# Two chained MLPs: VectorE writes the activations of an up tile into SBUF in place of PSUM

## The chip, the cores and the metric

The kernel runs on one core of one Trainium2 chip. The metric is the device time of one execution in microseconds, lower is better. TensorE, VectorE (DVE), ScalarE (ACT), GpSimd (POOL) and SyncE (SP) each run their own list of instructions in order and meet at semaphores.

## The reference

The input is 2 x 4096 rows of 192 features. A mixing stage weights 7 neighbouring rows with a softmax, and then two MLPs follow, each 192 to 2048 to 192, without a bias:

```python
x = attn_out.reshape(B * S, D)          # softmax-weighted sum of 7 rows, per head
h = x @ w_in                            # first MLP: 192 -> 2048
g = np.maximum(0.01 * h, h)             # leaky ReLU
x = g @ w_out                           # 2048 -> 192
h = x @ w_in2                           # second MLP
g = np.where(h > 0.0, h, np.exp(np.minimum(h, 0.0)) - 1.0)   # ELU
out = g @ w_out2
```

All of it is in float32.

## The kernel before

**Numbers in two parts.** TensorE multiplies in the rounded type fp32r. To keep float32 precision each factor is split into a rounded part (`_hi`) and the rest (`_lo`), and three of the four products are made. ScalarE makes the rounded part with a copy that converts, and VectorE makes the rest with a subtraction.

**Tiles.** The 8192 rows are cut into 16 chunks of 512 rows (`T`). A phase is one MLP of one chunk. There are 32 of them, in the order of `run`: the first MLP of chunk c, the second MLP of chunk c-1, and so on. So the two MLPs alternate (m is 0 in the first, 1 in the second; c is the chunk; ph counts the phases; dm and dc name the phase before, whose down still runs). A phase has 8 steps (s; g counts them over all phases). A step makes 256 of the 2048 hidden features: two halves of 128 features by 512 rows, side by side in a tile of 128x1024.

**One step on its way through the engines:**
- TensorE, `up`: ten matmuls into `hidden[:, s % 2, :]`, in PSUM (two buffers of two banks). The semaphore `s_up` counts it.
- ScalarE writes `act[:, s % 2, :]`, in SBUF: 0.01 times hidden in the first MLP (L762); relu(-hidden), then exp of its negative, in the second (L765, L767). `s_act`.
- VectorE, `nonlinearity`: the maximum of the two, written back over `hidden` in PSUM (L894 in the first MLP, L897 in the second). `s_g`.
- ScalarE rounds it: `hid_hi` from `hidden` (L792). `s_hi`.
- VectorE takes the rest: `hid_lo` = `hidden` - `hid_hi` (L933). `s_lo`.
- TensorE, `down`: ten matmuls of `hid_hi` and `hid_lo` with the down weights `dn` into `y_a` and `y_b` (L524 to L531). `s_dn`.

`hidden`, `act`, `hid_hi` and `hid_lo` have two buffers each, chosen by s % 2. TensorE's order is up of step g, down of step g-2, up of g+1, down of g-1. Before up of step g it waits for `hid_lo` of step g-2 (`s_lo`), since that is the last reader of the PSUM buffer. Down of g-2 then needs no wait of its own.

**Work beside this.** GpSimd makes the mixing of a later chunk, `mixing`, from chunk 1 on: 7 products and 6 additions of 128x768, all from SBUF to SBUF (L281, L293). It starts when VectorE has finished the softmax weights of that chunk, in step 2 of a first-MLP phase. ScalarE and VectorE also split the inputs of a phase (L693, L695 and L858, L860 in steps 3 and 4 of a first-MLP phase; L677, L679 and L849, L851 in steps 5 and 6 of a second-MLP phase), transpose mixed and output chunks in 32x32 squares (L879, L889), and take y out of PSUM: in step 1 of a phase ScalarE copies y of the phase before (`ylow` and `ya`) and VectorE adds into `yb` (L874). TensorE waits for both (`s_ya`, `s_yb`) before the first down of the new phase, in step 2. In the first phases they also split the weights of both MLPs (L814, L341, L342).

The very first and the very last step are cut into halves (`step_by_halves`), with the same sequence.

Of the kernel before, what the change touches and what calls it, by code (L numbers as in the profile page):

```python
# [5 lines left out]
def attention_leaky_elu_mlps(  # L6
# [24 lines left out]
    f32 = mybir.dt.float32  # L31
    f32r = mybir.dt.float32r
    ALU = mybir.AluOpType
    ACT = mybir.ActivationFunctionType
# [31 lines left out]
    with ctx:  # L66
# [45 lines left out]
        act = sb("act", [P, 2, 2 * T], f32)  # L112
        zeros = act[:, 0, 0:T]
        hid_hi = sb("hid_hi", [P, 2, 2 * T], f32r)
        hid_lo = sb("hid_lo", [P, 2, 2 * T], f32r)
# [8 lines left out]
        hidden = ps("hidden", [P, 2, 2 * T])  # L124
# [32 lines left out]
        s_g = sem("hidden_ready")  # L157
        s_hi = sem("hidden_hi_ready")
        s_lo = sem("hidden_lo_ready")
# [5 lines left out]
        s_hi1 = sem("half_hidden_hi_ready")  # L165
# [49 lines left out]
        END = ST * LAST + ST - 1  # L215
# [8 lines left out]
        def signal(step_sem, half_sem, i):  # L224

            return step_sem if i else half_sem
# [27 lines left out]
        def known(c):  # L254
            return isinstance(c, int)
# [39 lines left out]
        def down_split(m, n):  # L295

            parts = DN_PARTS * m + n + 1
            return (s_dnlo, parts) if parts <= DN_POOL else (s_dnlov, parts - DN_POOL)
# [189 lines left out]
        def _(pe):  # L488
# [104 lines left out]
            def phase(m, c, ph, dm, dc):  # L593
                for s in range(ST):
                    g = ST * ph + s
                    if known(ph) and g == 0:
                        up_first()
                        continue
                    if s == 0:

                        pe.wait_ge(s_min if m else s_xin, 2 * (c + 1))
                    if known(ph) and ph == 0 and s % 2 == 0:

                        pe.wait_ge(s_uplo, s + 2)
                    if known(ph) and ph == 2 and s == 0:

                        pe.wait_ge(s_uplo, 4 * QUARTERS)
                    if not (known(ph) and ph == 0 and s < 2):

                        pe.wait_ge(s_lo, g - 1)  # L610
                    up(m, input_of(m, c), g, s)
                    if known(ph) and ph in (0, 2) and s in (2, 4, 6, 7):

                        pe.wait_ge(*down_split(m, (s - 1) // 2))
                    if s < 2:
                        if dm is not None:
                            down(dm, ST - 2 + s)
                    else:
                        if s == 2 and dm is not None:

                            pe.wait_ge(s_ya, ph)
                            pe.wait_ge(s_yb, ph)
                        down(m, s - 2)
                    if s == 6 and known(ph) and ph == 0:
                        transpose_mix(1)
# [14 lines left out]
        def _(act_e):  # L640
# [83 lines left out]
            def step_by_halves(m, g, s):  # L724
                if g == END:

                    act_e.wait_ge(s_g, END - 1)
                for i in (0, 1):
                    wait_half(act_e, s_up, s_up1, g, i)
                    a, h = act[:, s % 2, HALF[i]], hidden[:, s % 2, HALF[i]]  # L730
                    if m == 0:
                        nc.scalar.activation(a, h, ACT.Copy, scale=SLOPE).then_inc(signal(s_act, s_act1, i), 1)
                    else:
                        nc.scalar.activation(a, h, ACT.Relu, scale=-1.0).then_inc(signal(s_relu, s_relu1, i), 1)
                        act_e.wait_ge(signal(s_relu, s_relu1, i), ST * CH if i else 1)
                        nc.scalar.activation(a, a, ACT.Exp, scale=-1.0).then_inc(signal(s_act, s_act1, i), 1)
                if g == 0:
                    softmax_exp(1)
                if g == END:

                    act_e.wait_ge(s_dn, END - 1)
                for i in (0, 1):
                    wait_half(act_e, s_g, s_g1, g, i)
                    nc.scalar.activation(hid_hi[:, s % 2, HALF[i]], hidden[:, s % 2, HALF[i]], ACT.Copy).then_inc(signal(s_hi, s_hi1, i), 1)

            def phase(m, c, ph, dm, dc):
                for s in range(ST):
                    g = ST * ph + s
                    if halved(g):
                        step_by_halves(m, g, s)  # L750
                        if g == 0:
                            round_up(0, 2)
                        continue
                    if known(ph) and ph == 0 and s == 7:
                        mlp1_input_hi(1, 0)
                        mlp1_input_hi(1, 1)
                    act_e.wait_ge(s_up, g + 1)
                    if not (known(ph) and ph == 0 and s < 2):

                        act_e.wait_ge(s_g, g - 1)  # L760
                    if m == 0:
                        nc.scalar.activation(act[:, s % 2, :], hidden[:, s % 2, :], ACT.Copy, scale=SLOPE).then_inc(s_act, 1)  # L762
                    else:

                        nc.scalar.activation(act[:, s % 2, :], hidden[:, s % 2, :], ACT.Relu, scale=-1.0).then_inc(s_relu, 1)  # L765
                        act_e.wait_ge(s_relu, ST * c + s + 1)
                        nc.scalar.activation(act[:, s % 2, :], act[:, s % 2, :], ACT.Exp, scale=-1.0).then_inc(s_act, 1)  # L767
                    if s == 1 and dm is not None:
                        take_y(dm, dc, ph - 1)
                    if m == 1 and s in (5, 6) and not (known(c) and c >= CH - 2):  # L770
                        mlp1_input_hi(c + 2, s - 5)
                    if m == 0 and s in (3, 4) and not (known(c) and c == 0):
                        mlp2_input_hi(c - 1, s - 3)
                    if known(ph) and ph == LAST - 1 and s in (3, 4):
                        mlp2_input_hi(CH - 1, s - 3)
                    if m == 0 and s == 1 and not (known(c) and c in (0, CH - 1)):
                        softmax_exp(c + 1)
                    if known(ph) and g == 1:
                        round_up(0, 3)
                    if known(ph) and g in (2, 3, 4):  # L780
                        round_down(0, DN_POOL + g - 2)
                    if known(ph):
                        if (ph, s) in UP2_AT:
                            round_up(1, UP2_AT.index((ph, s)))
                        if (ph, s) in DN2_AT:
                            round_down(1, DN2_AT.index((ph, s)))

                    act_e.wait_ge(s_g, g + 1)
                    if not (known(ph) and ph == 0 and s < 2):

                        act_e.wait_ge(s_dn, g - 1)
                    nc.scalar.activation(hid_hi[:, s % 2, :], hidden[:, s % 2, :], ACT.Copy).then_inc(s_hi, 1)  # L792

            softmax_exp(0)
            round_up(0, 0)
# [10 lines left out]
        def _(dve):  # L806
# [84 lines left out]
            def nonlinearity(m, h, a, done):  # L891
                if m == 0:

                    nc.vector.tensor_tensor(h, h, a, ALU.max).then_inc(done, 1)  # L894
                else:

                    nc.vector.scalar_tensor_tensor(out=h, in0=a, scalar=-1.0, in1=h, op0=ALU.add, op1=ALU.max).then_inc(done, 1)  # L897

            def step_by_halves(m, g, s):
                for i in (0, 1):  # L900
                    wait_half(dve, s_act, s_act1, g, i)
                    nonlinearity(m, hidden[:, s % 2, HALF[i]], act[:, s % 2, HALF[i]], signal(s_g, s_g1, i))
                for i in (0, 1):
                    wait_half(dve, s_hi, s_hi1, g, i)
                    nc.vector.tensor_tensor(hid_lo[:, s % 2, HALF[i]], hidden[:, s % 2, HALF[i]], hid_hi[:, s % 2, HALF[i]].bitcast(f32),
                                            ALU.subtract).then_inc(signal(s_lo, s_lo1, i), 1)

            def phase(m, c, ph, dm, dc):
                for s in range(ST):
                    g = ST * ph + s  # L910
# [7 lines left out]
                        mlp1_input_lo(1, 1)  # L918

                    dve.wait_ge(s_act, g + 1)  # L920
                    h = hidden[:, s % 2, :]
                    nonlinearity(m, h, act[:, s % 2, :], s_g)
                    if known(ph) and g == 1:
                        split_up(0, 2)
                    if s == 1 and dm is not None:
# [4 lines left out]
                        softmax_b(c + 1)  # L930

                    dve.wait_ge(s_hi, g + 1)
                    nc.vector.tensor_tensor(hid_lo[:, s % 2, :], h, hid_hi[:, s % 2, :].bitcast(f32), ALU.subtract).then_inc(s_lo, 1)  # L933
                    if m == 1 and s == 2 and not (known(c) and c >= CH - 2):
                        turn_mix(c + 2)
                    if m == 1 and s in (5, 6) and not (known(c) and c >= CH - 2):
# [55 lines left out]
```

## Time and profile before

| | us |
|---|---|
| median of 3 runs | 1211.51 (1210.0 to 1213.1) |
| profiled execution, span | 1212.5 |
| TensorE matmuls busy | 1186.3 (98%) |
| VectorE busy | 814.6 (67%) |
| ScalarE busy | 745.8 (62%) |
| GpSimd busy | 354.3 (29%) |

The profiled execution's only time is its span, from its first to its last instruction. Each engine's busy time is the sum over its instructions. A "chain of waits" follows the work that ended last back to what released it. A table by stretches gives each engine's busy time in a part of the span, and the granted TensorE clock (1.00 is full). In a timeline a row is one instruction with its start and duration, and in square brackets the idle time of its engine before it and what ended that.

### The profile page before, as it was taken

The page shows a single profiled execution, that of the slowest core. Times are in us where ns is not written, and L with a number is a line of the kernel's source. Part 1 is how long each engine was busy: PE and PEld are TensorE (multiplying, and loading weights), DVE is VectorE, ACT ScalarE, POOL GpSimd, SP SyncE. Part 2 cuts the span into 40 slices and gives each one's busy share as a digit, 9 for nine tenths or more (in the row PEclk, how much of TensorE's full clock was granted, in tenths as well). Part 3 has the DMA queues.
Part 4 walks back from the last instruction along what each step waited for, and adds up shares of the span by engine and source line. Part 5 has one row for each costly group of instructions (what it writes and reads, how often), then busy time and mean ns, then how long its engine had stood idle before and what let it go on. Part 6 is the DMA issues. An engine that isn't in the chain of part 4 may idle for free.

```text
span 1212.5 us, 14538 instructions
## 1 busy us (share of the span) xinstructions
PE 1186.3 (98%) x5208; PEld 973.8 (80%) x5208; DVE 814.6 (67%) x778; ACT 745.8 (62%) x815; POOL 354.3 (29%) x216
## 2 busy tenths in 40 slices
PE   6798999999999999999999999999999999999998
PEld 4586888888888888888888888888888888888887
DVE  6877675666757666675766757666675766756555
ACT  3465757656575665747656575665747656575675
POOL 4725051150703307051150703307051150700000
PEclk8999999999999999999999999999999999999999
DMA  8221102011120101102010120211002010110001
GB/s 193 75 84 37 26 27 76 27 49 26 39 62 26 62 30 58 26 26 75 26 49 26 39 62 26 62 33 55 26 32 70 26 49 26 39 26 26 14 16 37
DMA packets 42723, 54.24 MB, mean 45 GB/s; under 512 B 3733, under 2 KB 32531, under 8 KB 42193
## 3 DMA queue, kind: packets, MB, share of 16 engines
q1 hardware_dynamic: 42704, 54.00, 15.0%
q8 instruction: 11, 0.18, 0.1%
q14 instruction: 8, 0.06, 0.0%
HBM read 36.29 MB, written 17.69 MB: 45 GB/s over the span
## 4 chain that ended last, share of the span: by engine, by line
PE 91%; DVE 5%; DMA 2%; ACT 1%; SPq 0%; issue 0%; POOL 0%; ACTq 0%; POOLq 0%
PE hidden L495 46%; PE y_b L524 9%; PE y_b L525 9%; PE y_a L531 9%; PE y_a L529 9%; PE y_a L530 9%; DMA raw_d<-in_moe_w_out_dram 2%; DVE hid_lo L933 1%; DVE hidden L894 1%; ACT hid_hi L792 1%; DVE up_b_lo L814 1%; DVE up_a_lo L814 1%; DVE dn L342 0%; DVE dn L341 0%; DVE in_b L860 0%; DVE in_a_lo L858 0%
## 5 line engine op out<-in xcount | busy, mean ns | idle before, releaser
L933 DVE TENSOR_TENSOR hid_lo<-hidden,hid_hi 128x1024 fp32r<-128x1024 f32 x254 | 311.0, 1224 | 241.7 <-ACT hid_hi L792 241.7
L792 ACT ACTIVATE hid_hi<-hidden 128x1024 fp32r<-128x1024 f32 x254 | 260.8, 1027 | 328.8 <-DVE hidden L894 202.1
L897 DVE SCALAR_TENSOR_TENSOR hidden<-act,hidden 128x1024 f32<-128x1024 f32 x129 | 157.5, 1221 | 100.2 <-ACT act L767 98.1
L281 POOL TENSOR_TENSOR mix<-xw,wk 128x768 f32<-128x768 f32 x15 | 23.3, 1551 | 685.8 <-DVE wk L840 683.3
L495 PE MATMUL hidden<-in_a_hi,up_a_hi 128*128 128x512 f32 x510 | 201.3, 395 | 12.4 <-DVE hid_lo L933 11.5
L524 PE MATMUL y_b<-hid_hi,dn 128*128 128x512 f32 x512 | 199.5, 390 | 1.3 <-DVE dn L342 1.3
L525 PE MATMUL y_b<-hid_lo,dn 128*128 128x512 f32 x512 | 199.4, 389 | 0.0
L495 PE MATMUL hidden<-in_a_hi,up_a_lo 128*128 128x512 f32 x510 | 199.3, 391 | 0.0
L495 PE MATMUL hidden<-in_a_lo,up_a_hi 128*128 128x512 f32 x510 | 199.2, 391 | 0.0
L529 PE MATMUL y_a<-hid_hi,dn 128*128 128x512 f32 x512 | 199.2, 389 | 0.0
L531 PE MATMUL y_a<-hid_lo,dn 128*128 128x512 f32 x512 | 199.2, 389 | 0.0
L530 PE MATMUL y_a<-hid_hi,dn 128*128 128x512 f32 x512 | 199.2, 389 | 0.0
L495 PE MATMUL hidden<-in_b,up_b_hi 128*128 128x512 f32 x510 | 199.1, 390 | 0.0
L495 PE MATMUL hidden<-in_b,up_b_lo 128*128 128x512 f32 x510 | 199.0, 390 | 0.0
L293 POOL TENSOR_TENSOR mix<-mix,prod 128x768 f32<-128x768 f32 x90 | 174.3, 1937 | 1.2
L894 DVE TENSOR_TENSOR hidden<-hidden,act 128x1024 f32<-128x1024 f32 (+1 forms) x129 | 156.6, 1215 | 25.0 <-ACT act L762 23.6
L762 ACT ACTIVATE act<-hidden 128x1024 f32<-128x1024 f32 x127 | 130.4, 1027 | 60.8 <-PE hidden L495 60.6
L281 POOL TENSOR_TENSOR prod<-xw,wk 128x768 f32<-128x768 f32 x90 | 145.5, 1623 | 4.7
L765 ACT ACTIVATE act<-hidden 128x1024 f32<-128x1024 f32 x127 | 130.7, 1029 | 21.7 <-PE hidden L495 13.3
L767 ACT ACTIVATE act<-act 128x1024 f32<-128x1024 f32 x127 | 134.6, 1060 | 4.0
L495 PEld LDWEIGHTS hidden<-in_a_hi,up_a_hi 128*128 128x128 f32 x510 | 96.0, 188 | 38.5 <-issue 12.6
L524 PEld LDWEIGHTS y_b<-hid_hi,dn 128*128 128x128 f32 x512 | 96.2, 188 | 21.7 <-DVE dn L342 1.7
(100 smaller groups left out, 1139.6 us busy)
## 6 DMA issues: line engine op xcount, KB each, us to landing
xw<-in_x_dram SPq DMA_DIRECT2D x14, 960.0 KB
raw_b<-squares_out SPq DMA_DIRECT2D x60, 96.0 KB, 2.2
out_dram<-staged SPq DMA_DIRECT2D x15, 384.0 KB, 2.3
squares_in<-prod SPq DMA_DIRECT2D x56, 96.0 KB, 2.0
squares_out<-ya SPq DMA_DIRECT2D x15, 256.0 KB, 2.0
raw_a<-squares_in SPq DMA_DIRECT2D x14, 256.0 KB, 2.8
raw_d<-in_moe_w_out_dram SPq DMA_DIRECT2D x2, 1536.0 KB, 14.1
raw_a<-in_moe_w_in_dram SPq DMA_DIRECT2D x2, 1024.0 KB, 9.1
```

The lines of the kernel that those rows point to most:

```text
L281: ops.tensor_tensor(dst, src, w, ALU.mult).then_inc(done, 1)
L293: ops.tensor_tensor(mix[:, j0:j1, :], mix[:, j0:j1, :], terms[k % n][:, j0:j1, :], ALU.add).then_inc(done, 1)
L495: last = nc.tensor.matmul(dst, w[m][:, cols], v[src][:, :], start=(n == 0), stop=(n == len(pairs) - 1))
L524: nc.tensor.matmul(y_b[:, :], dn[m][:, f, P:2 * P], hi, start=(f == 0), stop=False)
L525: return nc.tensor.matmul(y_b[:, :], dn[m][:, f, P:2 * P], lo, start=False, stop=(f == FT - 1))
L529: nc.tensor.matmul(y_a[:, :], dn[m][:, f, 0:P], hi, start=(f == 0), stop=False)
L530: nc.tensor.matmul(y_a[:, :], dn[m][:, f, 2 * P:3 * P], hi, start=False, stop=False)
L531: return nc.tensor.matmul(y_a[:, :], dn[m][:, f, 0:P], lo, start=False, stop=(f == FT - 1))
L792: nc.scalar.activation(hid_hi[:, s % 2, :], hidden[:, s % 2, :], ACT.Copy).then_inc(s_hi, 1)
L894: nc.vector.tensor_tensor(h, h, a, ALU.max).then_inc(done, 1)
L897: nc.vector.scalar_tensor_tensor(out=h, in0=a, scalar=-1.0, in1=h, op0=ALU.add, op1=ALU.max).then_inc(done, 1)
L933: nc.vector.tensor_tensor(hid_lo[:, s % 2, :], h, hid_hi[:, s % 2, :].bitcast(f32), ALU.subtract).then_inc(s_lo, 1)
```

## The change

VectorE's nonlinearity writes its result over `act` (SBUF) and no longer over `hidden` (PSUM). ScalarE's rounding and VectorE's subtraction read it there. `hidden` is then free once the nonlinearity is done, and `act` has to live until the subtraction is done. So three waits change. TensorE waits before up of step g for the nonlinearity of step g-2, and for `hid_lo` of step g-2 only between up of g and down of g-2. ScalarE waits before it writes `act` of step g for `hid_lo` of step g-2, where it waited for the nonlinearity. No instruction is added, removed or put in another place. In the list of `step_by_halves` the same is done for the two steps in halves.

```diff
@@ TensorE, phase
                     if not (known(ph) and ph == 0 and s < 2):
-                        pe.wait_ge(s_lo, g - 1)
+                        pe.wait_ge(s_g, g - 1)
                     up(m, input_of(m, c), g, s)
                     if known(ph) and ph in (0, 2) and s in (2, 4, 6, 7):
                         pe.wait_ge(*down_split(m, (s - 1) // 2))
+                    if not (known(ph) and ph == 0 and s < 2):
+                        pe.wait_ge(s_lo, g - 1)
@@ ScalarE, step_by_halves and phase
-                    act_e.wait_ge(s_g, END - 1)
+                    act_e.wait_ge(s_lo, END - 1)
...
-                    nc.scalar.activation(hid_hi[:, s % 2, HALF[i]], hidden[:, s % 2, HALF[i]], ACT.Copy)
+                    nc.scalar.activation(hid_hi[:, s % 2, HALF[i]], act[:, s % 2, HALF[i]], ACT.Copy)
...
-                        act_e.wait_ge(s_g, g - 1)
+                        act_e.wait_ge(s_lo, g - 1)
...
-                    nc.scalar.activation(hid_hi[:, s % 2, :], hidden[:, s % 2, :], ACT.Copy).then_inc(s_hi, 1)
+                    nc.scalar.activation(hid_hi[:, s % 2, :], act[:, s % 2, :], ACT.Copy).then_inc(s_hi, 1)
@@ VectorE, nonlinearity, step_by_halves and phase
-                    nc.vector.tensor_tensor(h, h, a, ALU.max).then_inc(done, 1)
+                    nc.vector.tensor_tensor(a, h, a, ALU.max).then_inc(done, 1)
...
-                    nc.vector.scalar_tensor_tensor(out=h, in0=a, scalar=-1.0, in1=h, op0=ALU.add, op1=ALU.max)
+                    nc.vector.scalar_tensor_tensor(out=a, in0=a, scalar=-1.0, in1=h, op0=ALU.add, op1=ALU.max)
...
-                    nc.vector.tensor_tensor(hid_lo[:, s % 2, HALF[i]], hidden[:, s % 2, HALF[i]], hid_hi[:, s % 2, HALF[i]].bitcast(f32),
+                    nc.vector.tensor_tensor(hid_lo[:, s % 2, HALF[i]], act[:, s % 2, HALF[i]], hid_hi[:, s % 2, HALF[i]].bitcast(f32),
...
-                    nc.vector.tensor_tensor(hid_lo[:, s % 2, :], h, hid_hi[:, s % 2, :].bitcast(f32), ALU.subtract).then_inc(s_lo, 1)
+                    nc.vector.tensor_tensor(hid_lo[:, s % 2, :], act[:, s % 2, :], hid_hi[:, s % 2, :].bitcast(f32), ALU.subtract).then_inc(s_lo, 1)
```

## Rows read from the trace of the kernel before

**Rows 1.** The page's chain that ended last: shares of the span by engine.
```profile
PE 91%; DVE 5%; DMA 2%; ACT 1%; SPq 0%; issue 0%; POOL 0%; ACTq 0%; POOLq 0%
```

**Rows 2.** Stretches: length, busy PE, PEld, DVE, ACT, POOL, clock, DMA share, GB/s.
```profile
29.00:112.00 83.00, 69.73 (x293) 54.88 (x294) 68.42 (x65) 41.48 (x53) 48.25 (x26) 0.98 0.22 65
164.00:1037.00 873.00, 873.00 (x3847) 720.66 (x3846) 586.27 (x554) 546.95 (x590) 269.18 (x157) 1.00 0.14 43
```

**Rows 3.** Waits: who waited for whom, us in total, times, longest.
```profile
PE hidden L495 <- DVE hid_lo L933: 11.5, 8, 2.8
```

**Rows 4.** TensorE: ten up matmuls in the chain, and a first up's timeline row.
```profile
630.41 2.27 PE hidden L495 x10
...
657.45 0.47 PE L495 MATMUL hidden<-in_a_hi,up_a_hi 128*128 128x512 f32 x1
```

**Rows 5.** Timeline of VectorE, one period: start, us, line, names, idle before.
```profile
672.95 1.22 DVE L933 TENSOR_TENSOR hid_lo<-hidden,hid_hi 128x1024 fp32r<-128x1024 f32 x1
...
677.01 1.22 DVE L933 TENSOR_TENSOR hid_lo<-hidden,hid_hi 128x1024 fp32r<-128x1024 f32 x1 [1.09 <-ACT hid_hi L792]
678.15 2.03 DVE L858 TENSOR_TENSOR in_a_lo<-ya,in_a_hi 128x512 fp32r<-128x512 f32 x1
680.10 1.22 DVE L894 TENSOR_TENSOR hidden<-hidden,act 128x1024 f32<-128x1024 f32 x1
...
683.67 1.89 DVE L860 TENSOR_TENSOR in_b<-yb,in_b 64x512 fp32r<-64x512 f32 x1
...
687.81 1.23 DVE L933 TENSOR_TENSOR hid_lo<-hidden,hid_hi 128x1024 fp32r<-128x1024 f32 x1 [1.10 <-ACT hid_hi L792]
688.95 0.97 DVE L889 STREAM_TRANSPOSE staged<-raw_b 128x768 f32<-128x768 f32 x1
...
704.14 0.68 DVE L874 TENSOR_TENSOR yb<-y_b,ylow 64x512 f32<-64x512 f32 x1
```

**Rows 6.** Groups by line: ScalarE's rounding at 128x512, from SBUF and from PSUM.
```profile
L693 ACT ACTIVATE in_a_hi<-ya 128x512 fp32r<-128x512 f32 x16 | 9.9, 622 | 0.0
...
L677 ACT ACTIVATE in_a_hi<-turn 128x512 fp32r<-128x512 f32 x2 | 1.2, 585 | 0.0
```

**Rows 7.** Timeline of GpSimd, the same period; L281 a product, L293 an addition.
```profile
673.27 1.55 POOL L281 TENSOR_TENSOR mix<-xw,wk 128x768 f32<-128x768 f32 x1 [49.88 <-DVE wk L840]
...
677.78 1.85 POOL L293 TENSOR_TENSOR mix<-mix,prod 128x768 f32<-128x768 f32 x1
679.71 1.88 POOL L281 TENSOR_TENSOR prod<-xw,wk 128x768 f32<-128x768 f32 x1
...
684.98 2.30 POOL L293 TENSOR_TENSOR mix<-mix,prod 128x768 f32<-128x768 f32 x1
...
692.28 3.78 POOL L293 TENSOR_TENSOR mix<-mix,prod 128x768 f32<-128x768 f32 x2
```

**Rows 8.** The tile in_a_lo: count, ns minimum/median/maximum, first and last start.
```profile
L858 DVE TENSOR_TENSOR in_a_lo<-ya,in_a_hi x16: 682/2028/2029, 91.9 to 1151.4; 128x512 fp32r<-128x512 f32 x16
L849 DVE TENSOR_TENSOR in_a_lo<-raw_a,in_a_hi x14: 681/682/683, 143.3 to 1087.9; 128x512 fp32r<-128x512 f32 x14
L849 DVE TENSOR_TENSOR in_a_lo<-turn,in_a_hi x2: 682/687/692, 23.1 to 66.0; 128x512 fp32r<-128x512 f32 x2
```

**Rows 9.** Two early TensorE stalls, and the stretches behind them, columns as above.
```profile
36.04 0.50 PE L495 MATMUL hidden<-in_a_hi,up_a_hi 128*128 128x512 f32 x1 [1.75 <-DVE hid_lo L933]
...
57.34 0.76 PE L495 MATMUL hidden<-in_a_hi,up_a_hi 128*128 128x512 f32 x1 [2.60 <-DVE hid_lo L933]
...
36.00:41.00 5.00, 4.83 (x20) 3.68 (x20) 4.20 (x3) 0.77 (x1) 4.92 (x4) 1.00 0.19 38
57.30:61.40 4.10, 4.06 (x11) 3.29 (x12) 3.01 (x4) 1.03 (x1) 0.00 (x0) 0.59 0.44 99
```

More of the change, by code:

```diff
@@ L743, in step_by_halves @@
                     wait_half(act_e, s_g, s_g1, g, i)
-                    nc.scalar.activation(hid_hi[:, s % 2, HALF[i]], hidden[:, s % 2, HALF[i]], ACT.Copy).then_inc(signal(s_hi, s_hi1, i), 1)
+                    nc.scalar.activation(hid_hi[:, s % 2, HALF[i]], act[:, s % 2, HALF[i]], ACT.Copy).then_inc(signal(s_hi, s_hi1, i), 1)
             def phase(m, c, ph, dm, dc):
@@ L892, in nonlinearity @@
                 if m == 0:
-                    nc.vector.tensor_tensor(h, h, a, ALU.max).then_inc(done, 1)
+                    nc.vector.tensor_tensor(a, h, a, ALU.max).then_inc(done, 1)
                 else:
-                    nc.vector.scalar_tensor_tensor(out=h, in0=a, scalar=-1.0, in1=h, op0=ALU.add, op1=ALU.max).then_inc(done, 1)
+                    nc.vector.scalar_tensor_tensor(out=a, in0=a, scalar=-1.0, in1=h, op0=ALU.add, op1=ALU.max).then_inc(done, 1)
             def step_by_halves(m, g, s):
@@ L920, in phase @@
                     dve.wait_ge(s_act, g + 1)
-                    h = hidden[:, s % 2, :]
-                    nonlinearity(m, h, act[:, s % 2, :], s_g)
+                    nonlinearity(m, hidden[:, s % 2, :], act[:, s % 2, :], s_g)
                     if known(ph) and g == 1:
```

## The prediction

> **What bounds the kernel now.** I read the chain of waits first. It is TensorE for 91% [rows 1]. The table by stretches then says where TensorE is the bound. From 164 to 1037 us it is busy for all of the 873 us at a full clock, and from 29 to 112 us it is busy for 69.7 of 83 us [rows 2]. The missing 13.3 us of that early stretch are mostly one wait: the list of waits puts 11.5 us, in 8 pieces, on the up matmuls standing behind VectorE's `hid_lo` [rows 3]. So in the long middle a gain on VectorE or ScalarE is worth nothing. A loss there costs nothing either, until it is larger than the slack. The prediction is therefore about slack, and about what makes a VectorE instruction longer.
>
> The slack comes from the timeline of one period: a phase of the first MLP (8 steps) and one of the second. Ten matmuls take 2.27 us, and a step is ten of up and ten of down, so 4.53 us. The phase that I walk through starts its first up at 657.45 [rows 4]. Up of step s starts at about 657.5 + 4.53 s, and down of step s starts when up of step s+2 has ended, 9.07 us after up of s ended. Before the change `hid_lo` of step s had to be there one up earlier, 6.8 us after up of s ended. For step 5 that is 689.2, and `hid_lo` ended at 687.81 + 1.23 = 689.04 [rows 5]. The margin is 0.2 us at the tightest step. The other tight place is the second MLP's step 2, where down waits for y of the phase before: due at 657.5 + 10 x 4.53 + 2.27 = 705.1, and the add into `yb` ended at 704.14 + 0.68 = 704.82 [rows 5], a margin of 0.3 us.
>
> **The waits that move.** Up now waits for the nonlinearity of step s-2 and no longer for its `hid_lo`. Down waits for `hid_lo` itself. That gives `hid_lo` 2.27 us more, and asks the nonlinearity by 6.8 us after its up, where it comes 2.3 to 3.4 us after it in an undisturbed step. ScalarE's write of `act` now waits for `hid_lo` of two steps before. That ends about when, or before, the nonlinearity of the step between has been rounded, and ScalarE is at that rounding until then, so I cost it at nothing (it would show as a ScalarE wait on L935). In the early stretch the later deadline alone could take back up to 2.3 us of each burst of stalls. VectorE is busy for 68.4 of the 83 us there [rows 2], so most stalls only move: worth 2 us by my reckoning, at most the 11.5 us of [rows 3].
>
> **ScalarE.** `hid_hi` is read from SBUF in place of PSUM. The same rounding at half the width took 622 ns from SBUF and 585 ns from PSUM [rows 6]: 0.04 us more an instruction, in a loop of the second MLP that has 0.1 us to spare in a step of 4.53. It costs nothing by itself.
>
> **VectorE, alone.** The nonlinearity's operands (one in PSUM, one in SBUF) now write SBUF. That is exactly the form of the old `hid_lo`, which took 1.22 to 1.23 us also while GpSimd ran [rows 5, 7]. So it stays at 1.22. The new `hid_lo` has both inputs in SBUF. Its nearest row is the 128x512 subtraction of the input: 681 to 683 ns with both inputs in SBUF, 682 to 692 ns with one in PSUM [rows 8]. So no gain: 1.22. The Trainium skill ("VectorE: DVE Perf Modes", the section on the TRN2 errata) gives SBUF sources a fixed cost 62 cycles lower than PSUM sources, which would be an estimated 0.065 us for each of 254; the rows of this case do not show it, and in a stretch where VectorE isn't the bound it would leave the time alone.
>
> **VectorE beside GpSimd. This is the term that decides.** The same subtraction with both inputs in SBUF (L858) has a median of 2028 ns, against 682 for L849, of the same size and form [rows 8]. What differs is GpSimd: L858 runs while GpSimd mixes. At 678.15 GpSimd was in an instruction that had begun at 677.78 and takes 1.85 us. VectorE's took 2.03, that is, it waited 1.35 us for GpSimd's to end and then ran its 0.68. At 683.67 the next one took 1.89, a wait of 1.2. GpSimd is held up too: its addition at 684.98, queued behind that one, took 2.30 and not 1.85, and the product at 679.71 took 1.88 and not the usual 1.55 [rows 5, 7]. Instructions with one input in SBUF don't wait: the old `hid_lo` took 1.23 within GpSimd's work, the transpose 0.97. So the rule that I read off: a VectorE instruction with two SBUF inputs and a GpSimd instruction exclude each other, whole instruction by whole instruction. After the change every `hid_lo` is such an instruction. By the Trainium skill ("SBUF — State Buffer", the section Who interferes with whom) this is an exclusive lock on a read interface that the two engines share, taken by a VectorE instruction with two SBUF inputs; the trace agrees, by the 2028 against 682 ns.
>
> GpSimd mixes from 673.27 to 696.07 in each period [rows 7], of 16 steps or 72.6 us. It does so 13 times from 164 us on: its 157 instructions up to 1037 us [rows 2] are 12 mixings of 13 and the first of another. Twice more it mixes in the early stretch. An added wait lies between 0 and one GpSimd instruction, 1.85 us. I walk the period. VectorE holds the lock 1.07 us for 1024 elements and 0.54 for 512, GpSimd 1.5 for a product and 1.8 for an addition.
> - `hid_lo` 2 runs at 672.95, so mixing starts at 674.0, not 673.27; its products end at 675.5, 677.0 and 678.5.
> - `hid_lo` 3 is ready at 677.03, an instant after the third product took the lock: waits 1.5, ends 679.75 (before: 678.24). L858 waits for the addition that had queued: 681.3 to 682.0. The nonlinearity of 4 then starts at 681.9 (before 680.10).
> - `hid_lo` 4 ready 684.3, waits 0.9, ends 686.4. L860 waits 1.4, ends 688.4. Nonlinearity 5 ends 689.5; up of step 7 wants it at 689.2. **Stall 0.3.**
> - `hid_lo` 5 ready 690.7, waits 1.0, ends 692.9; down of 5 was due at 691.5 + 0.3. **Stall 1.1.**
> - `hid_lo` 6 ready 696.1, waits 0.1. `hid_lo` 7 ready 699.7, waits 1.25, ends 702.2: **0.2** more. Mixing ends at 701.1, 5 us later than before, still ahead of VectorE's transpose of it, which comes after the add into `yb` of 704.14.
> - The second MLP starts late: its first nonlinearity at 702.1, the second at 706.4, behind relu and exp on ScalarE, and only then the add into `yb`, done at 708.3. Down was due at 705.1 + 1.6. **Stall 1.6.**
>
> Sum: 0.3 + 1.1 + 0.2 + 1.6 = 3.2 us a period. The same walk with the old `hid_lo` gives a stall of 0.1 where the trace has none, so I take 3.0. In 13 periods: **39 us**. After the last of them there is no mixing, so nothing is added.
>
> The early stretch: GpSimd is busy there for 48.3 us [rows 2], and a step takes some 6 us (83 us for 14 of them), so eight `hid_lo` fall into it, at a mean wait of 0.9 us (half a GpSimd instruction) on an engine whose work is the path: 7 us, less the 2 us of the later deadline. **+5 us**, between 0 and +10.
>
> Sum: 1212.5 (span of the profiled execution) + 39 + 5 = 1256.5; that execution's span stands 1.0 us above the median of 1211.5, so **1255 us**.
>
> **The ends of the range.** The walk hangs on who wins at 677.0, by 0.02 us. If `hid_lo` 3 wins, its 1.5 us fall away, and with them the nonlinearity of 5 is in time: some 1.2 us a period are left, 16 us in 13. With the early 5 that is 1232. If instead the waits at steps 6 and 7 are both long, the carry into the second MLP grows by one half instruction, 0.9: 3.9 a period, 51 + 5, so 1267.
>
> **Rivals.**
> - *The exclusion is there, but the races fall well:* 1232, or, with nothing in the early stretch, 1228. For it: one race within 0.02 us. Against: all the others have to fall well again after each shift. 22%.
> - *TensorE's clock falls in the new stalls.* After the stall of 2.60 us before 57.34 the granted clock is 0.59 and ten matmuls take 4.07 us and not 2.27, with the clock at 1.2 GHz for most of them; after the 1.75 us before 36.04 it stays at 1.00 [rows 9]. Were it to fall in each period, that is 1.8 x 13 = 23 us more, less what the slower matmuls give VectorE to catch up: up to 1278. My stalls are 1.1 and 1.6 us, on the side of the 1.75. 10%.
> - *The exclusion does not touch it, and the kernel gets faster:* if the long L858 came from something else (its source `ya`, say, just written by ScalarE), `hid_lo` stays at 1.22 and only the early stalls shrink. 2 us by the deadline, up to 10 if they vanish: 1210 to 1201. It decides from the point that no `hid_lo` inside mixing takes over 1.3 us. Against: GpSimd's own instructions are lengthened next to L858, and L858's shortest is 682 ns, at a time without mixing. 5%.
> - *The waits are there and slack swallows them* (the 2.27 us more): within 0.3% of now, 1208 to 1215. It needs the lag to stay below 2.3 us at step 5, and 0.3 at the add into `yb`, which the moved waits don't relax. 3%.
>
> The forecast itself: 60%. **Range** 1228 to 1274: it takes in the forecast, the well-fallen races and most of the clock case. About 0.3% (3.6 us) is what a measurement here can tell from nothing: faster by more 4%, within 4%, slower 92%.
>
> **What would show it.** In the profile after: `hid_lo` with mean above 1224 ns (five in 16 wait about 0.95, and the two early mixings likewise, so some 1500), and values of 1.3 to 3 us inside mixing, 1.22 outside; GpSimd's busy time up from 354 by 4 to 5 us a mixing, to 410 to 430; TensorE idle 1 to 4 us in each period of about 75.7 us, behind `hid_lo` in down (L524) near the end of the first MLP's phase, and behind the add into `yb` in the second MLP's step 2. The nonlinearities stay at 1.22 and `hid_hi` is at 1.06. Wrong would be: `hid_lo` at 1.22 throughout (then I misread the exclusion), or long `hid_lo` with TensorE at 873 of 873 (then I misread the slack), or granted clocks below 1 in the periods.

## The result and the profile after

| | us |
|---|---|
| median of before, beside it | 1212.3 (1210.0 to 1213.7) |
| median of after | 1233.7 (1232.2 to 1234.3) |
| ratio | 1.017 (95% interval 1.015 to 1.019) |
| profiled execution of after, span | 1232.5 |

The change makes the kernel 21.4 us slower. The forecast had the sign and the mechanism, and 1255 us for the time, which is twice the loss (43 us). 1233.7 is close to the 1232 that it gave its rival "the races fall well".

In the page, the busy rows of VectorE and GpSimd have grown, from 814.6 and 354.3 us before, though not one instruction was added:

```profile
PE 1195.8 (97%) x5208; PEld 975.7 (79%) x5208; DVE 858.3 (70%) x778; ACT 751.2 (61%) x815; POOL 431.3 (35%) x216
...
L935 DVE TENSOR_TENSOR hid_lo<-act,hid_hi 128x1024 fp32r<-128x1024 f32 x254 | 348.5, 1372 | 248.6 <-ACT hid_hi L795 248.6
L795 ACT ACTIVATE hid_hi<-act 128x1024 fp32r<-128x1024 f32 x254 | 269.4, 1061 | 366.4 <-DVE act L897 239.9
```

`hid_lo` has a mean of 1372 ns, where the page of before has 1224. `hid_hi` is at 1061 ns, against 1027. The list of waits shows what TensorE now stands behind (who, for whom: us in total, times, longest):

```profile
PE y_b L524 <- DVE yb L877: 10.7, 13, 0.8
...
PE hidden L495 <- DVE act L897: 6.0, 4, 2.8
...
PE y_b L524 <- DVE hid_lo L935: 3.5, 3, 2.3
...
PE y_b L524 <- DVE dn L342: 2.4, 1, 2.4
```

The first row is the new one: 13 times, once in each period, where [rows 2] had TensorE busy without a gap. In the timeline of TensorE one such gap is this:

```profile
718.28 0.39 PE L495 MATMUL hidden<-in_a_lo,up_a_hi 128*128 128x512 f32 x1
719.50 0.47 PE L524 MATMUL y_b<-hid_hi,dn 128*128 128x512 f32 x1 [0.83 <-DVE yb L877]
```

The gap is 0.83 us, but it costs more. From start to start the two matmuls lie 1.22 us apart, where a tenth of 2.27 us is usual, so 0.99 us are lost here and some 0.1 more in the next few starts.

The timeline of VectorE and then of GpSimd in one period, which answers to [rows 5] and [rows 7] (L861 and L863 are the old L858 and L860, L897 the old L894, L877 the old L874):

```profile
686.33 1.22 DVE L935 TENSOR_TENSOR hid_lo<-act,hid_hi 128x1024 fp32r<-128x1024 f32 x1
...
690.40 1.23 DVE L935 TENSOR_TENSOR hid_lo<-act,hid_hi 128x1024 fp32r<-128x1024 f32 x1 [1.14 <-ACT hid_hi L795]
691.54 2.04 DVE L861 TENSOR_TENSOR in_a_lo<-ya,in_a_hi 128x512 fp32r<-128x512 f32 x1
...
695.84 2.16 DVE L935 TENSOR_TENSOR hid_lo<-act,hid_hi 128x1024 fp32r<-128x1024 f32 x1 [1.13 <-ACT hid_hi L795]
698.03 2.21 DVE L863 TENSOR_TENSOR in_b<-yb,in_b 64x512 fp32r<-64x512 f32 x1
...
702.63 1.92 DVE L935 TENSOR_TENSOR hid_lo<-act,hid_hi 128x1024 fp32r<-128x1024 f32 x1 [1.13 <-ACT hid_hi L795]
...
707.68 1.23 DVE L935 TENSOR_TENSOR hid_lo<-act,hid_hi 128x1024 fp32r<-128x1024 f32 x1 [1.13 <-ACT hid_hi L795]
...
711.17 2.05 DVE L935 TENSOR_TENSOR hid_lo<-act,hid_hi 128x1024 fp32r<-128x1024 f32 x1 [1.13 <-ACT hid_hi L795]
...
718.68 0.68 DVE L877 TENSOR_TENSOR yb<-y_b,ylow 64x512 f32<-64x512 f32 x1
```

```profile
686.66 2.31 POOL L281 TENSOR_TENSOR mix<-xw,wk 128x768 f32<-128x768 f32 x1 [45.50 <-DVE wk L843]
688.93 4.10 POOL L281 TENSOR_TENSOR prod<-xw,wk 128x768 f32<-128x768 f32 x2
693.00 2.30 POOL L293 TENSOR_TENSOR mix<-mix,prod 128x768 f32<-128x768 f32 x1
```

Steps 2 to 7 stand at 686.33, 690.40, 695.84, 702.63, 707.68 and 711.17. Steps 4, 5 and 7 wait 0.9, 0.7 and 0.8 us for GpSimd (the walk had 0.9, 1.0 and 1.25), and step 6 waits for nothing (0.1 in the walk). Step 3 is the difference: the walk had it wait 1.5 us, and it waits for nothing. GpSimd's third product waits for it instead (4.10 us for two products, 3.05 when nothing is in the way). That product by itself:

```profile
690.43 2.60 POOL L281 TENSOR_TENSOR prod<-xw,wk 128x768 f32<-128x768 f32 x1
```

Where the 20 us between the two spans are: the first chunk's input split in a second-MLP phase starts at 143.3 in before and at 148.9 in after, the last of the 14 at 1087.9 and 1107.9 (the second row is the old L849 of [rows 8]):

```profile
L861 DVE TENSOR_TENSOR in_a_lo<-ya,in_a_hi x16: 684/2038/2043, 96.8 to 1171.4; 128x512 fp32r<-128x512 f32 x16
L852 DVE TENSOR_TENSOR in_a_lo<-raw_a,in_a_hi x14: 684/684/685, 148.9 to 1107.9; 128x512 fp32r<-128x512 f32 x14
L852 DVE TENSOR_TENSOR in_a_lo<-turn,in_a_hi x2: 683/688/692, 23.9 to 70.6; 128x512 fp32r<-128x512 f32 x2
```

So 5.6 us are lost before the periods, and 14.4 in 13 periods: 72.66 us became 73.77, 1.11 more. The tail costs nothing. Of the 5.6 us, 0.8 are not the change's: the very first split of an input starts at 23.9 in after and at 23.1 in before [rows 8], ahead of the first `hid_lo`. That leaves 4.8.

### The profile page after: what moved, and what is told of

It is laid out like the page before. It is cut to its first block, busy times and chain, and to the rows that moved or that the text cites. A ratio compares the mean times of both kernels' runs of the same rounds, so it can differ in the third digit from the quotient of the medians.

```text
span 1232.5 us, 14546 instructions
## 1 busy us (share of the span) xinstructions
PE 1195.8 (97%) x5208; PEld 975.7 (79%) x5208; DVE 858.3 (70%) x778; ACT 751.2 (61%) x815; POOL 431.3 (35%) x216
## 4 chain that ended last, share of the span: by engine, by line
PE 57%; DVE 19%; ACT 11%; issue 10%; DMA 2%; SPq 0%; DVEq 0%; ACTq 0%; POOL 0%; POOLq 0%
PE hidden L495 28%; DVE act L897 7%; PE y_b L524 6%; PE y_a L529 6%; PE y_b L525 6%; PE y_a L530 6%; PE y_a L531 6%; ACT hid_hi L795 5%; DVE in_b L863 3%; DVE in_a_lo L861 2%; ACT act L770 2%; ACT act L768 2%; DVE hid_lo L935 2%; DMA raw_d<-in_moe_w_out_dram 2%; DVE act L900 1%
## 5 line engine op out<-in xcount | busy, mean ns | idle before, releaser
L935 DVE TENSOR_TENSOR hid_lo<-act,hid_hi 128x1024 fp32r<-128x1024 f32 x254 | 348.5, 1372 | 248.6 <-ACT hid_hi L795 248.6
L795 ACT ACTIVATE hid_hi<-act 128x1024 fp32r<-128x1024 f32 x254 | 269.4, 1061 | 366.4 <-DVE act L897 239.9
L281 POOL TENSOR_TENSOR mix<-xw,wk 128x768 f32<-128x768 f32 x15 | 34.0, 2266 | 632.4 <-DVE wk L843 629.7
L900 DVE SCALAR_TENSOR_TENSOR act<-act,hidden 128x1024 f32<-128x1024 f32 x129 | 156.5, 1213 | 71.3 <-ACT act L770 69.3
L293 POOL TENSOR_TENSOR mix<-mix,prod 128x768 f32<-128x768 f32 x90 | 202.1, 2245 | 1.2
L281 POOL TENSOR_TENSOR prod<-xw,wk 128x768 f32<-128x768 f32 x90 | 184.0, 2051 | 4.7
L897 DVE TENSOR_TENSOR act<-hidden,act 128x1024 f32<-128x1024 f32 (+1 forms) x129 | 155.8, 1208 | 22.9 <-ACT act L765 21.1
```

Of the source, the lines that this page charges most:

```text
L281: ops.tensor_tensor(dst, src, w, ALU.mult).then_inc(done, 1)
L293: ops.tensor_tensor(mix[:, j0:j1, :], mix[:, j0:j1, :], terms[k % n][:, j0:j1, :], ALU.add).then_inc(done, 1)
L795: nc.scalar.activation(hid_hi[:, s % 2, :], act[:, s % 2, :], ACT.Copy).then_inc(s_hi, 1)
L897: nc.vector.tensor_tensor(a, h, a, ALU.max).then_inc(done, 1)
L900: nc.vector.scalar_tensor_tensor(out=a, in0=a, scalar=-1.0, in1=h, op0=ALU.add, op1=ALU.max).then_inc(done, 1)
L935: nc.vector.tensor_tensor(hid_lo[:, s % 2, :], act[:, s % 2, :], hid_hi[:, s % 2, :].bitcast(f32), ALU.subtract).then_inc(s_lo, 1)
```

## The experiments

The theory: a VectorE instruction with two SBUF inputs and an instruction of GpSimd exclude each other, and all of the loss is that. Rivals: the moved waits cost it; ScalarE's slower read from SBUF costs it. The second question is why the loss is half of the forecast: one lost or won race (`hid_lo` of step 3), or stalls overrated throughout.

**e1, GpSimd's mixing cut to next to nothing in the kernel after.** It leaves out all of the mixing but 24 of 768 columns.

```diff
-            heads = slice(j0 * H, j1 * H)
+            heads = slice(j0 * H, j0 * H + 1)
...
-                ops.tensor_tensor(mix[:, j0:j1, :], mix[:, j0:j1, :], terms[k % n][:, j0:j1, :], ALU.add).then_inc(done, 1)
+                ops.tensor_tensor(mix[:, j0, 0:GROUP], mix[:, j0, 0:GROUP], terms[k % n][:, j0, 0:GROUP], ALU.add).then_inc(done, 1)
```

(and the products of one head in the same way).

> The kernel after, with GpSimd's 13 mixing instructions of a chunk cut to one head of one row (24 of 768 columns), so that they hold nothing for long. This leaves most of the mixing out, and the result is not the reference's. Exclusion theory (VectorE's hid_lo, with both inputs in SBUF, and GpSimd's instructions shut each other out): all hid_lo at 1.22 us, no TensorE stall in the periods, 1200 to 1206 us, since the early waits behind GpSimd go as well. Theory that the moved waits cost the time (up behind the nonlinearity, ScalarE behind hid_lo): still 1225 to 1233. Theory that ScalarE's slower read of SBUF (1061 against 1027 ns) costs it: 1225 to 1233.

Measured: 1194.9 us (1194.3 to 1195.4), ratio to before 0.986 (0.984 to 0.988). That is faster than before and faster than the theory's 1200 to 1206. The moved waits and ScalarE's reads are all in there, so neither costs the time by itself. Of the moved waits, TensorE's is tested by this run alone, since e3 puts it back. The size was a miss: I had overlooked how much of the early stretch is GpSimd's in the kernel before as well. TensorE's waits for VectorE are gone altogether; the table of 25 to 112 us (columns as in [rows 2]), in e1 and then in before:

```profile
25.00:112.00 87.00, 86.94 (x386) 71.47 (x386) 67.07 (x81) 59.48 (x73) 12.52 (x28) 1.00 0.23 71
```

```profile
25.00:112.00 87.00, 73.39 (x310) 57.56 (x309) 71.97 (x71) 45.16 (x59) 50.29 (x28) 0.98 0.23 68
```

The 386 matmuls in place of 310 in the same time are what GpSimd's mixing takes from the start of both kernels. This run can't tell how much of it is exclusion and how much is that the first mixing is ready sooner.

**e3, the second SBUF input taken away.** `hid_lo` reads `hidden` again, so TensorE's wait before up has to be the one of before too; all else is as in after. The kernel leaves the nonlinearity out of what `hid_lo` is taken from.

```diff
-                        pe.wait_ge(s_g, g - 1)
+                        pe.wait_ge(s_lo, g - 1)
...
-                    nc.vector.tensor_tensor(hid_lo[:, s % 2, :], act[:, s % 2, :], hid_hi[:, s % 2, :].bitcast(f32), ALU.subtract).then_inc(s_lo, 1)
+                    nc.vector.tensor_tensor(hid_lo[:, s % 2, :], hidden[:, s % 2, :], hid_hi[:, s % 2, :].bitcast(f32), ALU.subtract).then_inc(s_lo, 1)
```

> The kernel after, with hid_lo reading the up tile in PSUM in place of act in SBUF, so that it has one SBUF input, and with TensorE's up again behind hid_lo (the tile is its input). The nonlinearity still writes SBUF, hid_hi still comes from there, ScalarE still waits for hid_lo before it writes act. hid_lo is then taken from the up tile before the nonlinearity, and the result is not the reference's. Exclusion theory: hid_lo at 1.22 us throughout, 1211 to 1215 us, as before. Theory of the waits or of ScalarE's reads: 1225 or more.

Measured: 1213.9 us (1210.9 to 1215.7), ratio 1.001 (1.000 to 1.002): before's time. VectorE writes SBUF, ScalarE reads it there and waits for `hid_lo`, and none of that costs anything. TensorE's waits are before's, row for row of [rows 3]:

```profile
PE hidden L495 <- DVE hid_lo L935: 11.5, 8, 2.8
```

The early loss is gone with it: from the first split of an input (20.9) to the marker of the periods (141.1) e3 takes 120.2 us, before takes 120.2 (23.1 to 143.3), and after 125.0 (23.9 to 148.9).

So the cost is in the two SBUF inputs of `hid_lo`. e1 shows that it needs GpSimd's work, e3 that it needs the second SBUF input.

**e2, the race of step 3, first attempt.** A small memset on VectorE ahead of that `hid_lo`.

```diff
                     dve.wait_ge(s_hi, g + 1)
+                    if m == 0 and s == 3:
+                        nc.vector.memset(nudge[:, :], 0.0)        # nudge: 128x8
```

> The kernel after, with a memset of 8 columns on VectorE between its wait for hid_hi and hid_lo, in step 3 of the first MLP's phases alone. In the profile after, that hid_lo starts 4.07 us behind the start of hid_lo of step 2 and takes 1.23 us, and GpSimd's third product then takes over 2 us: VectorE won by some 0.04 us. Theory of the race (the forecast's size was wrong because this one race went the other way): a delay of 0.06 to 0.1 us turns it, this hid_lo takes 2.6 to 2.75 us, a period grows by 1.5 to 2 us, the time is 1250 to 1258. Theory that the forecast overrated every stall and the race does not matter: 1233 to 1236, the memset alone being at most 0.1 us x 15 = 1.5.

> The kernel before with the same memset in the same place, as a control of its own cost. Theory of the race: there is no race to lose there, since hid_lo has one SBUF input, so 1211 to 1214 us (at most 0.1 us x 15 more). If the memset itself hurts, 1215 or more, and e2 has to be read against it.

Measured: 1231.6 us (e2) and 1212.3 us (e4, ratio 1.001, 1.000 to 1.002). No loss. But the timeline of e2 shows that the delay did not come about: `hid_lo` of step 3 starts 4.08 us behind that of step 2 (683.68), and 4.07 in after. The memset ran in time in which VectorE waited anyway. Inconclusive, then, and e4, with the same memset, says as little.

```profile
687.76 1.21 DVE L939 TENSOR_TENSOR hid_lo<-act,hid_hi 128x1024 fp32r<-128x1024 f32 x1 [1.15 <-issue]
687.78 0.07 DVE L938 MEMSET nudge<- 128x8 f32 x1
```

**e5, the same with 128 columns.**

> As the last one on the kernel after, with a memset of 128 columns in place of 8. The one of 8 columns fell into the time in which VectorE waited anyway: that hid_lo started 4.08 us behind the one of step 2, against 4.07, and still took 1.21, so the race was not turned. 128 columns should move it by 0.1 to 0.2 us. Theory of the race: hid_lo of step 3 waits for the rest of GpSimd's product, 1.5 us less the delay, so it ends at the same instant whatever the delay is; 2 us more a period, 1255 to 1262 us, the same within 2 us as with 768 columns. Theory that the race does not matter: 1232 to 1237.

Measured: 1233.1 us (1232.6 to 1234.3), ratio 1.017. Now the delay is real: `hid_lo` starts at 688.44, which is 4.20 us behind that of step 2 at 684.24. Still it took 1.16 us. GpSimd's third product waited, though its row starts at 688.33, 0.11 us before VectorE's: it took 2.68 us and not 1.55. VectorE and GpSimd in e5:

```profile
688.36 0.17 DVE L938 MEMSET nudge<- 128x128 f32 x1 [1.19 <-ACT hid_hi L796]
688.44 1.16 DVE L939 TENSOR_TENSOR hid_lo<-act,hid_hi 128x1024 fp32r<-128x1024 f32 x1
```

```profile
688.33 2.68 POOL L282 TENSOR_TENSOR prod<-xw,wk 128x768 f32<-128x768 f32 x1
```

So my picture of the race was off: VectorE can still get in when the row of GpSimd's next instruction has already begun. (e6, a memset of 768 columns, gave no run: its tile needs 3072 bytes of SBUF in each partition, and 608 were free. The next two delays are reductions over a constant tile, with a few columns of output.)

**e7 and e8, delays of 0.46 and 1.13 us, and e9, the longer one in the kernel before.**

```diff
                     dve.wait_ge(s_hi, g + 1)
+                    if m == 0 and s == 3:
+                        nc.vector.reduce_max(nudge[:, 0:3], ident[:, :].unsqueeze(1).broadcast_to((P, 3, P)), AX_X)   # e8, e9: 8
```

> The kernel after, hid_lo of step 3 in the first MLP's phases delayed by a reduction of 384 columns on VectorE (some 0.4 us, one SBUF input). With 128 columns it started 4.20 us behind hid_lo of step 2 and still went ahead of GpSimd's third product, so the port is free for at least 0.13 us between two products. Theory of the race, with a free gap of 0.15 to 0.3 us between two of GpSimd's instructions: 0.4 us falls behind the gap, hid_lo waits 1.0 to 1.2 us, a period grows by 1.5 to 2 us, 1252 to 1262 us. Theory that this race does not decide the size (VectorE's next instruction, L861, absorbs the delay, since it has to wait for GpSimd anyway): 1232 to 1237.

> The same with 1024 columns, some 1.1 us. Theory of the race: the delay lies inside the wait, hid_lo ends at the same instant as with 384 columns, 1252 to 1262, within 2 us of it. Theory of absorption: 1232 to 1237, or more by what sticks out, up to 0.5 us x 13.

> The kernel before with the same reduction of 1024 columns, the control of the delay by itself. There hid_lo has no race; behind it L858 waits for GpSimd to the same instant (1.35 us of wait in the profile before), so the 1.1 us are taken out of that wait: 1211 to 1214. If the delay adds to the chain: 1220 to 1226 (1 us x 13).

Measured: e7 1256.8 us (1254.6 to 1258.9), e8 1257.9 (1257.6 to 1258.9), e9 1213.3 (1211.1 to 1213.9; ratio 1.000, 0.999 to 1.001). The race is turned: against the before measured beside them (1213.6 us) the loss is 43.2 and 44.3 us, where after had 21.4. A delay more than twice as long costs the same, within 1.1 us. In the kernel before, the same delay costs nothing. VectorE in e7, and GpSimd:

```profile
700.38 2.19 DVE L939 TENSOR_TENSOR hid_lo<-act,hid_hi 128x1024 fp32r<-128x1024 f32 x1
702.49 2.32 DVE L862 TENSOR_TENSOR in_a_lo<-ya,in_a_hi 128x512 fp32r<-128x512 f32 x1
704.74 1.21 DVE L898 TENSOR_TENSOR act<-hidden,act 128x1024 f32<-128x1024 f32 x1
```

```profile
699.94 1.55 POOL L282 TENSOR_TENSOR prod<-xw,wk 128x768 f32<-128x768 f32 x1
```

`hid_lo` waits 1.0 us, the third product takes its undisturbed 1.55, and L862 then waits 1.6 us for an addition. In e8 `hid_lo` starts 0.67 later in its step and takes 1.52 us, 0.67 less, so it ends at the same instant. What TensorE waits for in e7 are the two main stalls of the forecast:

```profile
PE y_b L525 <- DVE yb L878: 18.2, 14, 1.4
PE y_b L525 <- DVE hid_lo L939: 10.8, 16, 1.9
```

The marker of the periods runs from 146.0 to 1128.3 in e7, so a period is 75.56 us, 2.90 more than before. The forecast's walk had 3.2, taken as 3.0; its stall of 0.3 us behind the nonlinearity of step 5 is not among e7's gaps in a period.

**Cutting GpSimd's instructions in two.** If exclusion is by whole instructions, then shorter ones make shorter waits. Each product and addition of the mixing is made in two pieces of 128x384:

```diff
             def product(k):
-                src = xw[:, k + j0:k + j1, :].rearrange("p j (h g) -> p (j h) g", h=H)
+                for a, b in pieces:          # (0, 2), (2, 4)
+                    src = xw[:, k + a:k + b, :].rearrange("p j (h g) -> p (j h) g", h=H)
...
+                for i, (a, b) in enumerate(pieces):
+                    eng.wait_ge(done, before + PIECES * (2 * k - 1) + i + 1)
+                    ops.tensor_tensor(mix[:, a:b, :], mix[:, a:b, :], terms[k % n][:, a:b, :], ALU.add).then_inc(done, 1)
```

> The kernel after, with every product and addition of GpSimd's mixing cut into two instructions of 128x384, so that a wait for it is at most half as long. Exclusion by whole instructions: hid_lo in mixing waits 0 to 0.9 us and not 0 to 1.9, the periods come back to 72.6 to 73 us, 1208 to 1216 us. If VectorE had to wait for a whole mixing or GpSimd took a share of the port's rate, cutting would change nothing: 1230 or more, GpSimd being longer by the fixed cost of 13 more instructions a chunk.

> The same cut in the kernel before. There only the splits of weights and inputs (two SBUF inputs) wait for GpSimd, and only in the first 112 us does TensorE wait for them in turn. Exclusion: the waits of up to 1.6 us there halve, 1202 to 1208 us, faster than both kernels. Else 1211 to 1214.

> The kernel before with GpSimd's products and additions cut into four instructions of 128x192. Waits for GpSimd are at most 0.5 to 0.7 us, but mixing is longer by the fixed cost of each instruction (some 0.25 us: 128x384 took 892 ns, 128x768 1550), 39 more a chunk, so 5 to 8 us a mixing more than with halves, and the first mixing, for which TensorE waits in the first phase, comes later. 1202 to 1208: as good as the halves or a little worse.

Measured: after with halves 1217.2 us (1215.0 to 1217.6), just above the 1208 to 1216 expected and 16 us better than after, ratio to before 1.003 (1.001 to 1.005). Before with halves 1202.8 us (1201.8 to 1203.6), ratio 0.992 (0.990 to 0.994), the fastest version that computes everything, about 10 us below before. Before with quarters 1206.5 us, ratio 0.994 (0.993 to 0.996); there TensorE waits 6.9 us for the first mixing, and 1.4 with halves. In after with halves the input split takes 1346 ns and not 2038, and the marker runs from 146.4 to 1091.0, a period of 72.66 us: the periods have lost nothing any more.

```profile
L864 DVE TENSOR_TENSOR in_a_lo<-ya,in_a_hi x16: 684/1346/1359, 93.4 to 1154.5; 128x512 fp32r<-128x512 f32 x16
L855 DVE TENSOR_TENSOR in_a_lo<-raw_a,in_a_hi x14: 683/684/684, 146.4 to 1091.0; 128x512 fp32r<-128x512 f32 x14
```

What is left between after with halves and before with halves (1217.2 and 1202.8) lies in the early stretch: the marker of the one starts at 146.4, of the other at 131.2. (1.7 us of it lie ahead of the first split of an input, at 23.7 and 22.0.) One row of the former's waits shows a part of the rest. GpSimd's first mixing takes from 31.3 to 63.3 us, where it takes from 29.4 to 56.6 in before with halves, and TensorE waits 5.4 us to transpose it (1.4 in the other). Being held up by `hid_lo` in its turn would do this to GpSimd:

```profile
PE turn L580 <- POOLq L472: 5.4, 1, 5.4
```

## Why the prediction was half right

**Slack, and where it ends.** Right. In the periods TensorE has one gap in after, behind the add into `yb` in step 2 of the second MLP's phase, one of the two places named as tight. The other one, `hid_lo` of step 5 ahead of down, shows in e7.

**The moved waits, ScalarE.** Right, by e1 and e3. ScalarE's rounding went from 1027 to 1061 ns, 0.034 us where 0.04 was taken, and no time followed. The gain in the early stretch that the moved deadline was to bring (2 us) was not measured by itself.

**VectorE alone.** Right. Outside mixing the new `hid_lo` has a median of 1226 ns, against 1225 in before. The nonlinearities are at a mean of 1208 and 1213 ns (1215 and 1221 in before), though they now write SBUF. The fixed gain of SBUF sources which the Trainium skill states ("VectorE: DVE Perf Modes", the section on the TRN2 errata) does not show at this form.

**VectorE beside GpSimd.** Right as a mechanism, by both directions: without GpSimd's work (e1) and without the second SBUF input (e3) the loss is gone, and shorter GpSimd instructions make shorter waits (the halves). The mean of `hid_lo` is 1372 ns and not some 1500, since three of them in a period wait and not five. GpSimd's busy time is 431 us, where 410 to 430 was forecast.

**The walk through the period is the step that failed.** It had 3.2 us, rounded to 3.0; measured 1.11. The line in it on `hid_lo` of step 3, "an instant after the third product took the lock: waits 1.5", is the mis-sized term. In after that `hid_lo` waits for nothing. The prediction named this race as the one on which the walk hangs, and put 1.2 us a period and 1232 us on its other outcome; 1.11 and 1233.7 were measured. With the race turned (e7, e8) the period grows by 2.90 us and the loss is 43 to 44 us, where the forecast said 43. So the walk's sum holds for the outcome that it assumed, and what went wrong was that outcome and its odds: 60% for losing and 22% for winning.

Two things were wrong behind these odds. The walk let the third product start 4.05 us behind `hid_lo` of step 2 (677.0 against 672.95), from a hold of VectorE of 1.07 us, which no row shows, and a round 1.5 us a product. In after it is 4.10 (690.43 against 686.33), and `hid_lo` of step 3, at 4.07, is 0.03 us ahead of it and not behind. And the walk let GpSimd hold the interface from the first moment of its row. e5 shows that it doesn't: VectorE's row came 0.11 us behind GpSimd's, and VectorE went first. In e7, 0.44 us behind (699.94 against 700.38), it waited. So with 0.03 us to either side `hid_lo` wins.

**The early stretch.** +5 forecast, 4.8 measured by the marker once the late start is taken off. That they agree is in part luck: of the sum's terms (eight waits of 0.9 us, less 2 for the later deadline) none was measured by itself. By e3 the second SBUF input is what costs it.

TensorE's clock falls here further than in before. In [rows 9] a stall of 1.75 us was followed by the full clock. In after, while the matmuls behind a stall of 2.25 us run, the clock falls to 1.2 GHz (a matmul takes 0.63 us from 39.59 on, where 0.39 is usual), and it is there still at 43.60 and 50.70:

```profile
38.22 0.50 PE L524 MATMUL y_b<-hid_hi,dn 128*128 128x512 f32 x1 [2.25 <-DVE hid_lo L935]
...
43.64 0.77 PE L495 MATMUL hidden<-in_a_hi,up_a_hi 128*128 128x512 f32 x1 [1.72 <-DVE act L897]
...
50.70 0.79 PE L524 MATMUL y_b<-hid_hi,dn 128*128 128x512 f32 x1 [2.45 <-DVE dn L342]
...
43.60:48.00 4.40, 4.36 (x10) 3.14 (x10) 3.38 (x2) 2.63 (x3) 4.32 (x3) 0.50 0.91 311
50.70:55.00 4.30, 4.30 (x10) 3.43 (x11) 3.17 (x3) 2.71 (x3) 4.22 (x3) 0.50 0.03 6
```

It costs next to nothing, as e2 shows, which is after but for a memset within a wait. From 29 to 56.4 us the granted clock is 0.88 on average in e2 and 0.69 in after. The same three stalls in e2:

```profile
35.86 0.50 PE L525 MATMUL y_b<-hid_hi,dn 128*128 128x512 f32 x1 [1.75 <-DVE hid_lo L939]
41.28 0.47 PE L496 MATMUL hidden<-in_a_hi,up_a_hi 128*128 128x512 f32 x1 [2.82 <-DVE act L898]
48.33 0.50 PE L525 MATMUL y_b<-hid_hi,dn 128*128 128x512 f32 x1 [3.23 <-DVE dn L343]
```

From the first of them to the third it is 12.47 us in e2 and 12.48 in after. At the lower clock TensorE works longer and waits less, since VectorE sets the time here. To the marker e2 takes 124.5 us (21.8 to 146.3), and after 125.0; that 0.5 is the most that the clock can have cost in this pair of executions. In the periods the granted clock stays at 1.00, so the rival of the clock falls.

## What to carry to other kernels

Before an operand moves from PSUM to SBUF, count the SBUF inputs of every VectorE instruction that reads it: with two of them, the instruction and GpSimd's work on SBUF wait for each other, instruction by instruction, and a busy GpSimd can make 1.22 us into 2 or more. If the two must run side by side, make GpSimd's instructions shorter; here two pieces in place of one gave 10 us to a kernel whose early waits had looked like part of the start. Four pieces gave 7. And where a hand-made schedule hangs on a race of a few hundredths of a microsecond, forecast both outcomes with like odds, since the trace's starts are not the instants at which the race is decided.

## What the runs showed of the hardware that I had not expected

The start of a GpSimd row is not the moment from which GpSimd shuts VectorE out: 0.11 us behind that start VectorE still went first (e5), 0.44 us behind it no longer (e7). The Trainium skill ("SBUF — State Buffer", the section Who interferes with whom) says "Issue order, not op shape, decides who blocks"; the runs agree that the one that comes second waits for the whole instruction, and show that the order can't be read off the starts of rows that lie 0.1 us apart. Where between 0.11 and 0.44 us the door closes was not measured. GpSimd's own fixed cost fits in there: by the medians a product of 128x384 took 865 ns and one of 128x768 took 1546, so about 0.2 us of an instruction does not grow with its columns. That the open time is this fixed part was not tested.

A lower TensorE clock can be free. For 17 us of the early stretch the granted clock was 0.50 in after, and the stalls behind it came as far apart as in e2, where it was 0.50 for 7 us: the matmuls filled time in which TensorE would have waited for VectorE.
